# The first block's loads between two DMA queues, and 15 warm-up products for 18

## The reference, cut to what matters

```python
# x, f_logit: (2, 6080, 256); lower_bound: (256,); w_in: (256, 2048); w_out: (2048, 256)
sig = 1 / (1 + exp(-f_logit))
f = lower_bound + (1 - lower_bound) * sig
h = 0
for t in range(6080):
    h = f[:, t] * h + (1 - f[:, t]) * x[:, t]
    y[:, t] = h
z = y.reshape(12160, 256) @ w_in
g = where(z > 0, z, exp(min(z, 0)) - 1)
out = g @ w_out
```

## Time and profile before

| | us |
|---|---|
| median of 3 runs | 961.0 (960.94 to 961.43) |
| the profiled execution, whole | 961.75 |
| its span, first to last instruction | 959.9 |
| TensorE busy in the span | 954.5 (99%) |
| first product that counts starts at | 8.47 |

### The profile page before, as it was taken

How to read it: one execution, slowest core, us unless ns; L and a number is a source line. 1 busy time by engine, 2 the same in 40 slices (tenths; PEclk the granted TensorE clock), 3 DMA queues, 4 the chain that set the end, 5 groups by cost and what they waited for, 6 DMA issues and landing times.

```text
span 959.9 us, 15015 instructions
## 1 busy us (share of the span) xinstructions
PE 954.5 (99%) x4362; PEld 815.6 (85%) x4362; DVE 722.9 (75%) x916; ACT 790.1 (82%) x1424; POOL 628.8 (66%) x475
## 2 busy tenths in 40 slices
PE   9999999999999999999999999999999999999998
PEld 6999888888888888888888888888888888888887
DVE  6998976976886796697688679678768867966444
ACT  7989888878888888888888888888888788887775
POOL 2588796576667668557656755856775765676544
PEclk9999999999999999999999999999999999999999
DMA  7212012002102201100210210120021021001001
GB/s 273 68 33 95 1 33 66 34 1 78 55 1 57 76 1 44 55 33 2 74 55 0 66 66 0 46 66 18 23 65 44 0 76 55 0 0 46 1 1 45
DMA packets 23078, 42.02 MB, mean 44 GB/s; under 512 B 2560, under 2 KB 4096, under 8 KB 23040
## 3 DMA queue, kind: packets, MB, share of 16 engines
q1 hardware_dynamic: 22752, 41.10, 13.2%
q10 hardware_dynamic: 288, 0.46, 0.2%
HBM read 29.10 MB, written 12.45 MB: 43 GB/s over the span
## 4 chain that ended last, share of the span: by engine, by line
PE 95%; ACT 2%; DVE 1%; issue 0%; DMA 0%; ACTq 0%; DVEq 0%
PE acc L893 17%; PE acc L895 17%; PE acc L894 17%; PE h L863 14%; PE h L865 14%; PE h L864 14%; ACT e L469 1%; PE h L998 1%; PE h L1000 1%; PE h L999 1%; ACT e L463 1%; DMA opening<-first_gate 0%; DVE x L625 0%; ACT opening L419 0%; PE h L964 0%
## 5 line engine op out<-in xcount | busy, mean ns | idle before, releaser
L335 POOL TENSOR_TENSOR g_lo<-e,g_hi 128x512 fp32r<-128x512 f32 (+1 forms) x384 | 516.6, 1356 | 325.2 <-ACT g_hi L477 323.8
L463 ACT ACTIVATE e<-h 128x512 f32<-128x512 f32 (+1 forms) x379 | 224.9, 594 | 124.3 <-PE h L865 90.1
L716 DVE SCALAR_TENSOR_TENSOR e<-e,h 128x512 f32<-128x512 f32 (+1 forms) x379 | 256.8, 677 | 70.2 <-ACT e L469 69.0
L893 PE MATMUL acc<-g_hi,w_out_hi 128*128 128x512 f32 (+1 forms) x768 | 291.1, 379 | 0.4 <-DVE w_out_lo L687 0.4
L895 PE MATMUL acc<-g_hi,w_out_lo 128*128 128x512 f32 (+1 forms) x768 | 291.0, 379 | 0.0
L894 PE MATMUL acc<-g_lo,w_out_hi 128*128 128x512 f32 (+1 forms) x768 | 290.9, 379 | 0.0
L469 ACT ACTIVATE e<-e 128x512 f32<-128x512 f32 (+1 forms) x384 | 241.2, 628 | 9.6 <-issue 1.1
L477 ACT CAST g_hi<-e 128x512 fp32r<-128x512 f32 (+1 forms) x384 | 232.0, 604 | 19.4 <-DVE e L716 19.4
L863 PE MATMUL h<-a_hi,w_in_hi 128*128 128x512 f32 x616 | 234.7, 381 | 0.0
L865 PE MATMUL h<-a_hi,w_in_lo 128*128 128x512 f32 x616 | 234.7, 381 | 0.0
L864 PE MATMUL h<-a_lo,w_in_hi 128*128 128x512 f32 x616 | 234.7, 381 | 0.0
(11 more groups left out here) (75 smaller groups left out, 555.8 us busy)
## 6 DMA issues: line engine op xcount, KB each, us to landing
opening<-forget_logit SPq DMA_DIRECT2D x44, 256.0 KB, 2.6
x<-value SPq DMA_DIRECT2D x44, 256.0 KB, 2.7
out<-out_sb SPq DMA_DIRECT2D x44, 256.0 KB, 2.0
w_in_raw<-w_in SPq DMA_DIRECT2D x8, 256.0 KB, 5.5
w_out_raw<-w_out SPq DMA_DIRECT2D x8, 256.0 KB, 6.6
out<-out_sb SPq DMA_DIRECT2D x4, 224.0 KB, 2.1
x<-value SPq DMA_DIRECT2D x3, 224.0 KB, 6.3
opening<-forget_logit SPq DMA_DIRECT2D x2, 224.0 KB, 6.4
```

Source lines behind the costliest of these rows:

```text
L335: nc.gpsimd.tensor_tensor(g_lo[:, t % RING, 0:w], e[:, t % TILES, 0:w], g_hi[:, t % RING, 0:w].bitcast(F32), ALU.subtract).then_inc(g_lo_r ...
L463: nc.scalar.activation(e[:, i, 0:w], bank_of(j, t)[:, 0:w], ACT.Relu, scale=-1.0).then_inc(r_ready, 1)
L716: nc.vector.scalar_tensor_tensor(e[:, t % TILES, 0:w], e[:, t % TILES, 0:w], -1.0, bank_of(j, t)[:, 0:w], ALU.add, ALU.max).then_inc(g_rea ...
L893: nc.tensor.matmul(bank, hi, g_h, start=opens, stop=False)
```

## The change

The diff is the whole change:

```diff
-WARM_UP = 18
+WARM_UP = 15
...
             sp.dma_start(opening[:, EDGE - HALVES:EDGE + SHORT], first_gate).then_inc(gate_loaded[0][0], 16)
-            load_x(0, 0, 0)
-            load_w_in(0)
+            load_gate(0, 0, 1)
             load_w_in(1)
             load_w_in(2)
             load_w_out(0)
...
-            act.dma_start(gate[:, 0, 1, 0:SHORT], forget_logit[0, :, 1, tokens(0)]).then_inc(gate_loaded[0][1], 16)
+            act.dma_start(x[:, 0, 0, 0:SHORT], value[0, :, 0, tokens(0)]).then_inc(x_loaded[0][0], 16)
+            act.dma_start(w_in_raw[:, 0, 0:4], w_in[0]).then_inc(w_in_loaded[0], 16)
             act.dma_start(x[:, 0, 1, 0:SHORT], value[0, :, 1, tokens(0)]).then_inc(x_loaded[0][1], 16)
```

## The result

The changed kernel takes 965.21 us, median of 15 runs (961.64 to 965.78), against 961.43 us for the kernel before over 15 runs taken with it. The ratio is 1.003 with a 95% interval of 1.0023 to 1.0036, so it is slower by 0.3%. (That is less than the quotient of the medians, 1.004, because a third of the changed kernel's runs lie near 962.) The forecast was 961.0, with 960.0 to 962.2 as its range: wrong, and outside the range.

The account below looks back on a forecast made before the run. TensorE, busy 954.5 of 959.9 us, was taken to bound the kernel, with the opening's start dates passing to the end. All terms were 0, so the forecast was the median of the runs shown, 961.0 us, range 960.0 to 962.2.

Parts of the forecast that it names:

- One more issue on ACT, term 0: ScalarE's opening: the third load's issue costs 0.45 us, table load ends at 3.4, tanh waits until 4.70; effect 0.
- Back to back from 11.48 us on: TensorE after the opening: products stand without gaps, so a shift in the opening passes to the program's end one for one.
- First gate: First load on SP's queue: lands at 4.67 as before, effect 0; bounds 1.3 us less or 0.2 us more.
- Second gate: Now second on SP's queue: lands at 5.5 instead of 4.85, covered until 5.9; effect 0, at worst 1.7 us lost.
- Second input and weights: Opening loads: input lands at 7.35, wanted at 7.74, at worst 0.3 us lost; weights no later than before; effect 0.
- Warm-up: TensorE's opening: 15 zero products end at about 7.5, idle grows from 0.31 to 0.95 us, real products start at 8.47; effect 0.
- The first rival: TensorE from 8.47 us: real products begin at 1.2 GHz, costing 2.0 us together, 963.0 us; chance 0.05.
- The rule of the Trainium skill that I weighed there: TensorE's clock: low by default, activity releases it, the rise moves between runs; so some shorter warm-ups might end before it.
- All the rivals: Opening: products at 1.2 GHz, 963.0, chance 0.05; a late load, 961.6, chance 0.12; `first_gate` sooner, 960.1, chance 0.04.

Follow-up runs that it names:

- the warm-up run: The kernel before with 15 zero products instead of 18, loads as before; 961.48 us, ratio 0.9996 (0.9986 to 1.0005).

## Why the prediction was wrong

**The step that failed is "One more issue on ACT, term 0".** I priced the third load by its 0.45 us of ScalarE's time at 1.7 us, which was right: the table load ended at 3.43 and tanh waited for its data until 4.41. I did not price its place in ScalarE's code. Every later ScalarE instruction moved by one against a fixed place in its instruction stream, where it stalls 880 us later. That the stall is the loading of code is inferred, from its fixed place and from the instruction packet ahead of its end in each trace; no run took the loading away. The run with one bare copy more and the run of the change with one wait less settle it from both sides (965.1 and 961.5). With the slot taken back, the forecast's sum of 0 is what was measured: 961.51, ratio 0.9999.

**The sum left out two terms** that follow from it: the pause of TensorE at 883 us, 0.2 us in the changed kernel's trace, and the pace behind it. Of the latter: 329 products start behind 884.1 us, on average 0.2307 us apart for 0.2200, 3.5 us. The pause and TensorE's lead of 0.22 us cancel, and 3.5 is what the span measured.

**Back to back from 11.48 us on** was not so. The starts of the products in the trace of before are 0.74 us apart at 45.7 us, 0.39 at 49.5, 0.37 at 52.2 and 0.51 at 66.5, where 0.193 is the pace. The list of waits shows only the first of them, because the rows are longer than the distance of their starts. That a shift passes on held even so: TensorE was 0.24 us ahead at 11.24 and 0.22 at 882.80.

**First gate.** The mechanism was right, the chain held link by link. It landed at 4.39 instead of 4.67, but that is scatter: with the old order of loads it took 3.38 us in the run with one copy more and 4.02 in the warm-up run, on either side of the 3.92 of the earlier trace rows. In the eight traces with the old order of these loads the first tanh starts at 4.15 to 4.79, in the six with the new order at 4.14 to 4.79. My bound above, 0.2 us, was right; below, up to 0.55 us come by chance with either order, and a date of one trace was taken for the kernel's.

**Second gate.** Forecast 5.5, found at 5.38 with the wait that was named; DVE's `weigh` and `scan` of half 1 followed without idle. In the run with the merged carry copy `first_gate` was earlier and the second gate landed at 5.6; there it set the chain. The margin of 0.4 us was about right.

**Second input and weights.** None was late: DVE had no wait for data and `round_plain(0)` ran at 6.75 (forecast 6.9).

**Warm-up.** The zeros ended at 7.4 (forecast 7.5), the idle was 0.80 (0.95), the products behind it 0.193 to 0.20 us apart, at 2.4 GHz. The first rival, a late rise of the clock, did not happen in the traces, and the warm-up run excludes it as a cost. The rule of the Trainium skill that I weighed there was beside the point, not contradicted.

**The chances.** Slower by over 0.2% had 0.05, for a reason that wasn't the one. All the rivals lay in the first 12 us, because the views that I read had been cut to them. The earlier trace rows held the general warning: where an engine is 99% busy, a pause anywhere counts, not only where the edit is. The trace of before did show the hole, 1.14 us with "issue" as its cause, and a margin of 0.28 us behind it.

The Trainium skill (Runtime: NRT & Kernel Launch, "Instruction fetch mechanics") has the matching rule: a sequencer takes its code in blocks, one ahead, and a branch breaks that order, so that the code wanted next may not be there. This case's trace agrees in kind, with the hole of 1.1 to 1.8 us behind the loop's end and the instruction packet ahead of its end; that the branch is its reason, no run here shows. The page calls the cost of crossing from one block to the next mostly hidden, and here it is hidden or costs 3.8 us by where one instruction falls.

## What to carry to other kernels

In this kernel one instruction more on ScalarE moved all its later code against a place where the engine stalls, ten microseconds behind a loop's end; whether other engines do it too was not tried. Look in the timeline behind each loop's end for idle with the cause "issue", and at the margin of what waits behind it; where that is TensorE, at the weight load's date and not the product's. A step that "costs nothing" in its own stretch should be measured with the count kept, by one harmless instruction more or less, before a result is put down to what was moved. And where times of one kernel fall into two groups, compare products per stretch, not busy shares: 274 against 261 in 60 us was the whole finding.

## What the runs showed of the hardware that was not expected

TensorE has two steady paces at the same granted clock: starts 0.220 or 0.230 us apart at 512 columns, 0.193 or 0.200 at 448. After a pause of some 0.9 us at 913 us it kept the slower one in six of six runs, after 0.2 to 0.3 us at the same place in one of eight, after a delay of about 0.1 us at 883 us in seven of twelve (the lengths are those of the profiled executions). The traces with a late copy behind 880 us keep it to their end.

It explains more than this change. The warm-up run's profiled execution took 1004.70 us, one of the times left out above, with the granted clock at full. It has the ordinary pause at 66.7 us, 0.2 us long, and after it the starts stay 0.20 us apart, and 0.23 at 512 columns:

```profile
66.71 0.44 PE L998 MATMUL h<-a_hi,w_in_hi 128*128 128x448 f32 x1
67.00 0.37 PE L999 MATMUL h<-a_lo,w_in_hi 128*128 128x448 f32 x1
67.20 0.36 PE L1000 MATMUL h<-a_hi,w_plain_lo 128*128 128x448 f32 x1
67.40 0.36 PE L998 MATMUL h<-a_hi,w_in_hi 128*128 128x448 f32 x1
```

```profile
800.00:880.00 80.00, 80.00 (x349) 1.00 0.13 39
```

That is 349 products in 80 us where the kernel before has 366. Behind 67 us 4,054 products start, at 0.0107 us more each 43.3 us; the execution is 43.2 us above the median of its kernel's compared runs. It is the only trace of such an execution.

The pause at 66 us mostly heals: the kernel before went back to 0.193 us within some ten products, the changed kernel too. Nor is the slower pace always kept: in the run of the change with one wait less it began at the pause of 51.8 us, and ended by itself at about 67. What holds the slower pace isn't settled; nothing in the rows names a releaser for it. Nor is it settled why five runs of the changed kernel end at 961.6 to 962.8.
